# Half of the down tiles of 18 units go through ScalarE and an adding DMA instead of VectorE

## What is computed

```python
# q, k, v: batch 2, heads 8, sequence 768, head size 64  ->  x: 1536 tokens x 512
state = gamma * state + outer(k[t], v[t]);  y[t] = scale * q[t] @ state

def _moe_ref(x, w_gate, w1, w2):        # 8 experts, hidden 1024
    P = exp(x @ w_gate - max)            # then 8 rounds of row and column normalisation
    for e in range(E):
        h = np.maximum(x @ w1[e], 0.0)
        out += P[:, e:e + 1] * (h @ w2[e])

def _moe2_ref(x, domain_probs, w1, w2):  # the same sum over 4 experts, gates given
```

## Time and profile before

| | |
|---|---|
| median of 3 runs | 1545.72 us (1545.34 to 1546.4) |
| profiled execution, first to last instruction | 1544.1 us |
| TensorE matmuls busy | 1538.1 us (100%) |
| VectorE busy | 880.1 us (57%) |
| ScalarE busy | 446.9 us (29%) |
| GpSimd busy | 49.5 us (3%) |
| DMA, mean over the span | 43 GB/s |

### The profile page before, as it was taken

How to read it: one execution, slowest core, us unless ns; L and a number is a source line. 1 busy time by engine, 2 the same in 40 slices (tenths; PEclk the granted TensorE clock), 3 DMA queues, 4 the chain that set the end, 5 groups by cost and what they waited for, 6 DMA issues and landing times.

```text
span 1544.1 us, 21412 instructions
## 1 busy us (share of the span) xinstructions
PE 1538.1 (100%) x8306; PEld 1396.6 (90%) x8306; DVE 880.1 (57%) x1419; ACT 446.9 (29%) x865; POOL 49.5 (3%) x45
## 2 busy tenths in 40 slices
PE   9999999999999999999999999999999999999999
PEld 8999989998999899989998999899998999899988
DVE  7756855555546455555565555576555556555553
ACT  5432322331223213222232132243331223213311
POOL 6100000000000000000000000012000000000000
PEclk9999999999999999999999999999999999999999
DMA  9100101101001011010010110101101001011011
GB/s 347 56 28 28 55 1 55 55 1 56 28 27 54 0 54 54 0 54 27 27 54 0 54 54 2 55 1 55 55 1 55 28 28 54 0 54 55 1 44 66
DMA packets 34458, 66.56 MB, mean 43 GB/s; under 512 B 2016, under 2 KB 2528, under 8 KB 34400
## 3 DMA queue, kind: packets, MB, share of 16 engines
q1 hardware_dynamic: 34256, 65.65, 12.3%
q10 hardware_dynamic: 144, 0.10, 0.0%
HBM read 62.59 MB, written 3.15 MB: 43 GB/s over the span
## 4 chain that ended last, share of the span: by engine, by line
PE 98%; DMA 1%; issue 0%; POOL 0%; SPq 0%; DVE 0%; POOLq 0%
PE banks L1220 17%; PE banks L1221 17%; PE banks L1219 17%; PE banks L1195 15%; PE banks L1199 15%; PE banks L1197 15%; DMA qt_in<-in_q_t 1%; PE banks L1159 0%; PE banks L1105 0%; DMA k_in<-in_k 0%; PE banks L1061 0%; POOL q_up L400 0%; PE banks L1079 0%; PE banks L1141 0%; PE banks L1139 0%
## 5 line engine op out<-in xcount | busy, mean ns | idle before, releaser
L1195 PE MATMUL banks<-x_hi,w_hi 128*128 128x384 f32 x1344 | 450.6, 335 | 0.0
L1199 PE MATMUL banks<-x_hi,w_lo 128*128 128x384 f32 x1344 | 450.3, 335 | 0.0
L1197 PE MATMUL banks<-x_lo,w_hi 128*128 128x384 f32 x1344 | 450.0, 335 | 0.0
L1221 PE MATMUL banks<-w_hi,h_lo 128*128 128x512 f32 x1148 | 448.3, 391 | 0.0
L1220 PE MATMUL banks<-w_lo,h_hi 128*128 128x512 f32 x1148 | 448.2, 390 | 0.0
L1219 PE MATMUL banks<-w_hi,h_hi 128*128 128x512 f32 x1148 | 447.6, 390 | 0.0
L917 DVE SCALAR_TENSOR_TENSOR acc<-banks,gate,acc 128x512 f32<-128x512 f32 x251 | 188.5, 751 | 372.5 <-PE banks L1221 372.5
L591 ACT COPY ups<-banks 128x384 f32<-128x384 f32 x288 | 138.0, 479 | 887.8 <-PE banks L1199 887.8
L869 DVE TENSOR_TENSOR ups<-banks,ups 128x384 f32<-128x384 f32 x288 | 155.6, 555 | 189.5 <-ACT ups L591 167.8
L1221 PEld LDWEIGHTS banks<-w_hi,h_lo 128*128 128x128 f32 x1148 | 215.6, 188 | 44.7
L1219 PEld LDWEIGHTS banks<-w_hi,h_hi 128*128 128x128 f32 x1148 | 215.8, 188 | 43.4
(11 more groups left out here) (105 smaller groups left out, 479.8 us busy)
## 6 DMA issues: line engine op xcount, KB each, us to landing
w_raw<-in_moe_w SPq DMA_DIRECT2D x46, 1024.0 KB, 5.0
kt_in<-in_k_t SPq DMA_DIRECT2D x12, 256.0 KB, 6.9
qt_in<-in_q_t SPq DMA_DIRECT2D x12, 256.0 KB, 8.3
v_in<-in_v SPq DMA_DIRECT2D x12, 256.0 KB, 8.5
k_in<-in_k SPq DMA_DIRECT2D x10, 256.0 KB, 8.8
out<-acc SPq DMA_DIRECT2D x2, 768.0 KB, 3.5
out<-acc SPq DMA_DIRECT2D x5, 256.0 KB, 2.0
w_raw<-in_moe_w SPq DMA_DIRECT2D x4, 256.0 KB, 9.6
```

The costliest lines, as they stand in the source:

```text
L1195: nc.tensor.matmul(o, w1_hi[:, w, kc, fs], x_hi[:, x, kc, at], start=start and kc == 0, stop=False, skip_group_check=True)
L1197: nc.tensor.matmul(o, w1_hi[:, w, kc, fs], x_lo[:, x, kc, at], start=False, stop=False, skip_group_check=True)
L1199: last = nc.tensor.matmul(o, w1_lo[:, w, kc, fs], x_hi[:, x, kc, at], start=False, stop=kc == 1, skip_group_check=True)
L1221: last = nc.tensor.matmul(o, h_lo[:, f, b, rows], w2_hi[:, f, :], start=False, stop=(n == UC - 1))
```

## The change

In units 3 to 14 and 17 to 22 (`is_staged`), tiles 0 to 2 of each pair are no longer added by VectorE. ScalarE multiplies the tile by the gate (a column of gates, copied to `gate_col` once for each unit) and writes it to a new buffer `staged` of three tiles. When the three are there, GpSimd issues one DMA that adds `staged` to the three rows of `acc` (768 KB). The semaphore `staged_out` counts the staged tiles, `added` the finished DMAs (16 each). There is one buffer `staged`, so the first staging of a pair waits for the DMA of the pair before. TensorE waits for `staged_out` before tiles 2 to 4 and for the add of tile 3 before tile 5. VectorE adds tiles 3 to 5 alone and counts 2 for each, so that the sums of `acc_written` stay the same. Line numbers of the changed kernel are higher: L509 to L516 are L539 to L546 there, L716 is L770, L917 is L970, the staging is L664, the DMA L476.

```diff
+STAGED_1, STAGED_2 = 3, 2 * E1 + 1
+STAGED_N1, STAGED_N2 = L1_LAST - STAGED_1, L2_LAST - STAGED_2
...
+        gate_col = sb("gate_col", [P, NSUB])
+        sb("place", [P, 36])
...
+            staged = sb("staged", [P, CPB, DM], F32, moe)
...
+        def is_staged(k):
+
+            return not isinstance(k, int) or STAGED_1 <= k < L1_LAST or STAGED_2 <= k < L2_LAST
+
+        def units_staged(k, layer):
+            return k - (STAGED_1 if layer == 1 else STAGED_2 - STAGED_N1)
+
+        def pairs_staged(k, p, layer):
+            return PAIRS * units_staged(k, layer) + p
...
+            def add_staged(n, p):
+                pool.wait_ge(staged_out, CPB * n + CPB)
+                pool.wait_ge(acc_scaled, 4 * CPB)
+                rows = acc[:, row_of(p, 0):row_of(p, CPB - 1) + 1, :]
+                pool.dma_start(rows, staged[:, :, :], accum_op=ALU.add).then_inc(added, 16)
+
+            pool.wait_ge(acc_written, downs_before(STAGED_1, 0))
+            for n in range(PAIRS * STAGED_N1):
+                add_staged(n, n % PAIRS)
...
             for n in range(CH, 2 * CH):
                 sums_low(n)
+            pool.wait_ge(acc_written, downs_before(STAGED_2, 0))
+            for n in range(PAIRS * STAGED_N1, PAIRS * (STAGED_N1 + STAGED_N2)):
+                add_staged(n, n % PAIRS)
...
+            def stage_out(k, p, n, gate, col, skip_added=False):
+                for u in range(CPB):
+                    act.wait_ge(down_done, downs_before(k, p) + (u + 1))
+                    if u == 0 and not skip_added:
+                        act.wait_ge(added, 16 * n)
+                    nc.scalar.mul(staged[:, u, :], down_bank[u % 2][:, :],
+                                  gate_col[:, row_of(p, u):row_of(p, u) + 1]).then_inc(staged_out, 1)
+
+            def staged_units(k, layer, gate, col):
+                if not isinstance(k, int) or k != STAGED_1:
+                    act.wait_ge(staged_out, CPB * pairs_staged(k, 0, layer))
+                for p in range(PAIRS):
+                    unit(k, p)
+                    if p == 0:
+                        nc.scalar.copy(gate_col[:, :].unsqueeze(2), gate[:, :, bass.ds(col, 1)]).then_inc(
+                            gate_col_ready, 1)
+                        act.wait_ge(gate_col_ready, units_staged(k, layer) + 1)
+                    stage_out(k, p, pairs_staged(k, p, layer), gate, col,
+                              skip_added=isinstance(k, int) and k == STAGED_1 and p == 0)
+                split_w1_high(k + 1, 0)
+                split_w1_high(k + 1, 1)
...
             units(2)
-            units(3)
+            act.wait_ge(acc_scaled, 4 * CPB)
+            staged_units(3, 1, gate1, 1)
             with act.Fori(2, E1 - 1) as e:
-                units(2 * e)
-                units(2 * e + 1)
-            units(L1_LAST - 1)
+                staged_units(2 * e, 1, gate1, e)
+                staged_units(2 * e + 1, 1, gate1, e)
+            staged_units(L1_LAST - 1, 1, gate1, E1 - 1)
...
+                nc.vector.memset(act_warm[:, 0:1], 0.0).then_inc(gate2_ready, 1)
...
+                if is_staged(k):
+                    nc.vector.scalar_tensor_tensor(a, y, gate[:, i, bass.ds(col, 1)], a,
+                                                   ALU.mult, ALU.add).then_inc(acc_written, 2)
+                elif how == "plain":
...
             def down(k, p, gate, col, how="add", split_next=False):
                 for u in range(2 * CPB):
-                    add_expert(k, p, u, gate, col, how)
+                    if u >= CPB or not is_staged(k):
+                        add_expert(k, p, u, gate, col, how)
                     if split_next and u < 4:
...
+            dve.wait_ge(added, 16 * PAIRS * STAGED_N1)
...
+            dve.wait_ge(added, 16 * PAIRS * (STAGED_N1 + STAGED_N2))
             down(L2_LAST, 0, gate2, E2 - 1)
...
+                    if staged is not None and CPB > u - 2 >= 0:
+                        pe.wait_ge(staged_out, CPB * staged + (u - 1))
+                    elif staged is not None and u == 2 * CPB - 1:
+                        pe.wait_ge(acc_written, downs_before(k, p) + 2)
+                    elif not (first and u < 2):
...
+            def staged_unit(k, layer):
+                for p in range(PAIRS):
+                    up(k, p)
+                    down(k, p, staged=pairs_staged(k, p, layer))
...
-            unit(3)
+            staged_unit(3, 1)
             with pe.Fori(2, E1 - 1) as e:
-                unit(2 * e)
-                unit(2 * e + 1)
-            unit(L1_LAST - 1)
+                staged_unit(2 * e, 1)
+                staged_unit(2 * e + 1, 1)
+            staged_unit(L1_LAST - 1, 1)
```

More of the change, by code:

```diff
@@ L110, in retention_moe_moe_kernel @@
         power_steps = small[:, (CH - 1) * HEADS + DC:].rearrange("p (w g) -> p w g", g=HEADS + DC)
-        sb("place", [P, 48])
+        gate_col = sb("gate_col", [P, NSUB])
+        sb("place", [P, 36])
         with ExitStack() as att:
@@ L216, in retention_moe_moe_kernel @@
         stored = sem("stored")
+        gate2_ready = sem("gate2_ready")
+        staged_out = sem("staged_out")
+        gate_col_ready = sem("gate_col_ready")
+        added = sem("added")
         out_d = out.rearrange("(i p) n -> p i n", p=P)
@@ L664, in _ @@
             split_w1_high(L1_LAST + 2, 1)
-            units(L1_LAST + 2)
+            act.wait_ge(gate2_ready, 1)
+            staged_units(L1_LAST + 2, 2, gate2, 0)
             with act.Fori(E1 + 1, E1 + E2 - 1) as e:
-                units(2 * e)
-                units(2 * e + 1)
-            units(L2_LAST - 1)
+                staged_units(2 * e, 2, gate2, e - E1)
+                staged_units(2 * e + 1, 2, gate2, e - E1)
+            staged_units(L2_LAST - 1, 2, gate2, E2 - 1)
             units(L2_LAST, split_next=False)
@@ L913, in add_expert @@
                 dve.wait_ge(acc_written, downs_before(k, p) + (u + 1 - 12))
-                if how == "plain":
+                if is_staged(k):
+                    nc.vector.scalar_tensor_tensor(a, y, gate[:, i, bass.ds(col, 1)], a,
+                                                   ALU.mult, ALU.add).then_inc(acc_written, 2)
+                elif how == "plain":
                     nc.vector.tensor_tensor(a, y, a, ALU.add).then_inc(acc_written, 1)
@@ L1201, in up, with down @@
                         last.then_inc(up_done, 1)
-            def down(k, p, first=False, x2=None, last_rows=False):
+            def down(k, p, first=False, x2=None, last_rows=False, staged=None):
                 if p == 0:
@@ L1211, in down @@
                         pe.wait_ge(logits_out, 1)
-                    if not (first and u < 2):
+                    if staged is not None and CPB > u - 2 >= 0:
[3 more added lines that the diff above has]
+                    elif not (first and u < 2):
                         pe.wait_ge(acc_written, downs_before(k, p) + (u - 1))
@@ L1273, in _ @@
             down(L1_LAST + 1, 1)
-            unit(L1_LAST + 2)
+            staged_unit(L1_LAST + 2, 2)
             with pe.Fori(E1 + 1, E1 + E2 - 1) as e:
-                unit(2 * e)
-                unit(2 * e + 1)
-            unit(L2_LAST - 1)
+                staged_unit(2 * e, 2)
+                staged_unit(2 * e + 1, 2)
+            staged_unit(L2_LAST - 1, 2)
             up(L2_LAST, 0)
```

## The result

The changed kernel takes 1566.72 us (median of 4 runs, 1566.23 to 1567.22) against 1545.8 us for the kernel before on the same chip: a ratio of 1.0135, 95% interval 1.0121 to 1.015. The loss of 20.9 us is almost four times the 5.6 us forecast, and the time lies outside the range.

A forecast was written before the change was run, and what follows sets the result against it. TensorE was taken as the bound, with 98% of the chain. The profiled span of 1544.1 us plus 5.6 us of stalls gave 1549.7, and 1.6 more for timed runs 1551.3 us; 8 in 10 range 1546.5 to 1560.

The forecast's parts named there:

- So TensorE runs at a fixed pace and waits for nobody: TensorE's 512-column matmuls start 0.227 us apart without a pause, so the change can only make TensorE wait.
- It comes 0.31 us late: Second pairs: VectorE's add of tile 3 ends 0.31 us after TensorE loads the first weights of tile 5.
- 18 units x 0.31: The tile 5 stall, once in each changed unit's second pair: 5.6 us in all, bounds 3.2 to 12.6.
- Worth nothing: Removing 108 adds of 0.75 us (81 us) from VectorE gains no time, as VectorE idles before such adds.
- Staging and DMA: ScalarE's multiplication of a tile takes 0.68 us, GpSimd's adding DMA about 6 us to landing; both hidden.
- What is late next: The last w_lo and SP's w2 load come 1.7 us later, within 6.0 us of slack before product 6.
- Rival 1: The tile 5 wait stays under 0.17 us, too small to measure: 1545.7 to 1548.8 us, chance 0.20.
- Rivals 2 and 3: Adding DMA collides with the w2 load (1564 us, chance 0.08); GpSimd's descriptor writing holds VectorE up (1560 us, 0.07).
- Rival 4: Faster, as disturbance of TensorE by VectorE's PSUM reads goes away; put at 1545 us, chance 0.03.

The follow-up runs named there:

- experiment 2: Changed kernel with `place` cut from 36 to 28 elements, so h_hi, h_lo, ups and acc start where they did in the kernel before: 1550.88 us, ratio 1.0032.
- experiment 11: Changed kernel with h at its old address and, in second pairs, VectorE's add of tile 3 behind all four w_lo: 1570.84 us, ratio 1.0161.
- experiment 8: Changed kernel with h at its old address and, in second pairs, VectorE's add of tile 3 ahead of the third w_lo: 1546.28 us, ratio 1.0003.
- Experiment 10: Kernel before with 32 bytes put in between x_lo and w1_hi, so w1, w2 and h move and x stays: 1542.95 us, ratio 0.9981.

## Why the prediction was wrong

**The step that failed** is "So TensorE runs at a fixed pace and waits for nobody". The pace was read correctly, 0.227 us in the earlier trace rows, and then treated as a property of the matmul. It hangs on the memory layout: 0.233 us in the changed kernel. The working went through every instruction and wait of the change and left out the two lines of it that only lay out memory, so that the whole of the loss, bar 0.6 us, stands in no term, and no rival has it either. From the first up matmul to the end the changed kernel takes 21.2 us more, all of it in down parts: 20.6 by the pace, 0.6 by the stalls. That is more than the 20.4 us between the spans because the attention ahead of the experts happened to be 0.8 us shorter in the profiled execution of the changed kernel (its first up matmul starts 43.2 us in, 44.1 before).

**"It comes 0.31 us late"**: right for the kernel it was computed for. With the layout of before the load is 0.32 us late (experiment 2). **"18 units x 0.31"** was mis-sized: some 0.1 us of lateness is absorbed. I took the start of the weight load as the moment of need, while the matmul of this load starts only 0.23 us later (605.63 and 605.86 in experiment 2). Measured 0.23 us a stall, 4.1 us in all, and one to one beyond that (experiment 11). In the changed kernel as it stands this term is 0.6 us.

**"Worth nothing"** for the 108 adds taken off VectorE: right. Its busy time falls from 880.1 to 797.7 us, and with both costs removed the time is that of before (experiment 8).

**Staging and DMA**: right, 0.689 us and 5.7 us to landing (6.7 at most); TensorE waits for neither. **What is late next**: right, nothing. SP issues the w2 load at 675.88, 15.3 us after the down part's first matmul (660.58), where it was 13.4 (604.25 and 590.89): 1.9 us later, of which 1.7 were forecast, and no wait before product 6 appears.

**Rival 1** (no stall that can be measured) is right about the stall in the changed kernel as it stands, by luck: the slower pace made the chain less late. Its time, 1545.7 to 1548.8 us, is as wrong as the forecast's. **Rivals 2 and 3** did not happen: the adding DMA lands within 6.7 us, the w2 load takes 5.1 us to landing as against 5.0, and no w_lo is stretched: the three take 2.88 us as computed, though GpSimd issues from 670.16 to 671.02, over the first 0.18 us of the first. By the Trainium skill (SBUF — State Buffer, section Who interferes with whom) nothing was to be added there. The trace agrees, as far as an overlap of 0.18 us can tell. **Rival 4** said that the fixed step leaves no room. Experiment 10 finds 3 us by 32 bytes, in the first matmuls of each part, so that was wrong as well, though not for the disturbance by VectorE that the rival named.

## What to carry to other kernels

Where TensorE is the bound, its pace is the first thing to compare between two kernels, before any wait: the distance between two starts in the same loop, or the length of a whole part. If it differs from the first matmul on, look at where the tiles lie, also when the diff seems to touch only a small tile elsewhere, and restore the distances between the tiles before judging the rest of the change. Here, taking 108 adds off VectorE, which waited for each of them, gave nothing, while the order of what stayed there cost 4.1 us.

## What the hardware showed that I had not expected

With matmuls of 512 columns in fp32r whose weights come from one SBUF tile while another is streamed, moving the one against the other by 32, 64 or 128 bytes costs 0.37 to 0.44 us on a down part of 16.36 us (2.3 to 2.7%), and by 256 bytes nothing; moving both together by 32 bytes costs nothing. With 384 columns (w1 loaded, x streamed), 64 and 128 bytes cost 0.25 and 0.16 us on 14.59, and 32 bytes nothing. The granted clock was 1.00 in all of these runs, and the weight load itself takes 187 or 188 ns in each. What in the memory makes this so was not tried. A weight load that comes 0.17 us late delays the work by 0.03 us, one that comes 0.32 us late by 0.23, and one that comes 1.45 us late by 1.37.
